# Two tiles of the first expert's early rows run beside the routing of the last batch, table look-ups moved ahead of a tile's waits, fewer zero rows stored late

## The reference, cut to what matters

```python
# attention: 4 batches x 8 heads = 32 heads, 576 rows, head size 64, with decay, causal
x = attention(q, k, v, f).transpose(...).reshape(2304, 512)
# mixture of 8 experts, each row goes to one expert
logits = normed(x) @ normed(expert_emb).T / tau
expert_idx, gate_w = argmax(logits), softmax(logits)[argmax]
for e in range(8):
    mask = expert_idx == e
    h = np.maximum(x[mask] @ w1[e], 0.0)             # 512 -> 1024
    out[mask] = gate_w[mask, None] * (h @ w2[e])     # 1024 -> 512
# dense part: w_in 512 -> 2048, softplus, w_out 2048 -> 512
out = softplus(out @ w_in) @ w_out
```

## Time and profile before

| | |
|---|---|
| median of 3 runs | 1006.88 us (1004.63 to 1007.55) |
| the profiled execution, its own time | 1005.88 us |
| its span, first to last instruction | 1004.0 us |
| mean granted TensorE clock | 0.976 of full |
| busy in the span | PE 950.3, DVE 564.8, ACT 399.2, POOL 321.3 us |

### The profile page before, as it was taken

One profiled execution on the slowest core, in us unless ns is written; L12 is line 12 of the kernel. 1 busy time (PEld: TensorE's weight loads), 2 busy tenths in 40 slices (PEclk: granted clock), 3 DMA queues, 4 the chain that ended last, 5 costly groups with the idle time before them and its releaser, 6 DMA issues.

```text
span 1004.0 us, 17301 instructions
## 1 busy us (share of the span) xinstructions
PE 950.3 (95%) x5536; PEld 827.0 (82%) x5537; DVE 564.8 (56%) x1153; ACT 399.2 (40%) x684; POOL 321.3 (32%) x169
## 2 busy tenths in 40 slices
PE   6999999999926999999999989999999999999997
PEld 4888888888815877887888778989989899899896
DVE  7566667787555556646666755344444434444433
ACT  6567667666431112302322133333333333333332
POOL 7355464353326334814777630010010100100101
PEclk9899999999968999999999999999999999999999
DMA  6664654484167153643666410010010000000000
GB/s 151 158 162 102 157 140 115 117 245 109 54 215 242 55 180 104 222 151 87 212 218 218 165 43 22 11 42 22 1 42 22 31 22 10 31 0 0 32 1 32
DMA packets 56011, 98.98 MB, mean 99 GB/s; under 512 B 23648, under 2 KB 23648, under 8 KB 55456
## 3 DMA queue, kind: packets, MB, share of 16 engines
q1 hardware_dynamic: 37440, 46.99, 17.9%
q10 hardware_dynamic: 15616, 41.96, 13.0%
q0 software_dynamic: 2912, 9.46, 2.5%
HBM read 81.14 MB, written 17.22 MB: 98 GB/s over the span
## 4 chain that ended last, share of the span: by engine, by line
PE 89%; DVE 5%; DMA 2%; issue 2%; POOL 1%; ACT 0%; POOLq 0%; DVEq 0%; SPq 0%; ACTq 0%
PE ps L1479 20%; PE ps L1492 19%; PE ps L1435 11%; PE ps L1414 11%; PE ps L1307 10%; PE ps L1268 7%; PE ps L1291 5%; PE ps L1324 2%; PE ps L1423 2%; DMA x_raw<-xs_dram 1%; DVE tile_meta L1131 1%; PE ps L1398 1%; PE ps L1269 1%; PE ps L1466 1%; DMA qk_raw<-qkT 0%
## 5 line engine op out<-in xcount | busy, mean ns | idle before, releaser
L1492 PE MATMUL ps<-W,ghl 128*128 128x512 f32 x864 | 215.4, 394 | 1.3 <-DVE ghl L1196 1.3
L522 POOL TENSOR_TENSOR W<-raw,W 128x2048 fp32r<-128x2048 f32 x36 | 165.2, 4615 | 141.7 <-ACT W L728 141.7
L1479 PE MATMUL ps<-yTh,W 128*128 128x384 f32 x768 | 198.7, 339 | 2.0 <-DVE yTl L1184 2.0
L1492 PEld LDWEIGHTS ps<-W,ghl 128*128 128x128 f32 x864 | 160.4, 188 | 32.1 <-DVE ghl L1196 1.6
L1190 DVE SCALAR_TENSOR_TENSOR sp_a<-ps,sp_a 128x384 f32<-128x384 f32 x96 | 53.5, 557 | 210.3 <-ACT sp_a L757 210.3
L728 ACT CAST W<-raw 128x2048 fp32r<-128x2048 f32 x36 | 67.1, 1909 | 222.5 <-PE ps L1414 88.9
L753 ACT ACTIVATE sp_a<-ps 128x384 f32<-128x384 f32 x96 | 47.3, 492 | 259.4 <-PE ps L1479 255.5
L1479 PEld LDWEIGHTS ps<-yTh,W 128*128 128x128 f32 x768 | 141.0, 189 | 9.2 <-issue 2.2
L557 POOL DMA_INDIRECT out<-out_sb,out_row x18 | 17.3, 960 | 380.9 <-DVE out_sb L1209 379.1
L1479 PE MATMUL ps<-yTl,W 128*128 128x384 f32 x384 | 130.1, 339 | 0.0
L1307 PE MATMUL ps<-v_ring,pT_sb 128*128 128x100 f32 (+1 forms) x960 | 119.5, 266 | 1.9 <-DVE lgh L867 1.9
(11 more groups left out here) (233 smaller groups left out, 1277.5 us busy)
## 6 DMA issues: line engine op xcount, KB each, us to landing
raw<-w ACTq DMA_DIRECT2D x28, 1024.0 KB, 6.5
qk_raw<-qkT SPq DMA_DIRECT2D x64, 288.0 KB, 4.5
x_raw<-xs_dram SPq DMA_DIRECT2D x22, 257.0 KB, 4.8
ys_dram<-y_sb SPq DMA_DIRECT2D x21, 256.5 KB, 5.9
y_raw<-ys_dram SPq DMA_DIRECT2D x18, 256.5 KB, 2.6
vT_ring<-vT SPq DMA_DIRECT2D x16, 288.0 KB, 4.4
v_ring<-v SPq DMA_DIRECT2D x32, 128.0 KB, 4.0
first_raw<-w ACTq DMA_DIRECT2D x4, 1024.0 KB, 5.6
```

The source lines that it names most:

```text
L522: pool.tensor_tensor(wcols(par, 1, c), RAW[c][:, :], wcols(par, 0, c).bitcast(F32), ALU.subtract).then_inc(wl_done, 1)
L1479: ins = pe.matmul(bank(f_ % 2, GN), W[:, a:a + P], y[par][:, c, :], start=(m == 0), stop=(m == 3 * DC - 1))
L1492: ins = pe.matmul(bank(2 + k), ghl[:, (f_ + 2) % 4, part, k * P:k * P + P], W[:, a:a + DM], start=(f_ == 0 and m == 0), stop=(f_ == FC2 - ...
```

## The change

1. **Early tiles.** Before the last batch is routed, SP loads the first 256 rows of expert 0's region into two buffers (`x_raws`). PE, DVE and ACT work them as tiles 0 and 1 with expert 0's weights. The rows' own tiles are taken out of the table: `early_rows` is the smaller of 256 and the rows that expert 0 has from the first three batches, and the remaining rows make tiles from 2 on. Tables and counts are longer by two. In these two tiles ACT, not DVE, takes the relu and the high part of the hidden values, and ACT scales the result of tile 0.
2. **Order on PE.** The two tiles' products are written in pieces among `ranks(LAST)` and the turns, in other PSUM banks. Half products of w1 have 12 matmuls, and w2 is cut into 12 + 12 for tile 0 and 12 + 6 + 6 for tile 1. The loop begins at tile 3.
3. **Look-ups.** All four look-ups of a pass of PE's loop stand at its head.
4. **Zeros.** Two zero stores for the first 256 rows are made near the start, ahead of the scatters. Late ones follow as before, but all seven others now stand ahead of `load_x(3)` in SP's queue.
5. 32 instead of 24 warm-up matmuls at the start. DVE's table code has a few more short operations.

The core of the diff (the rest is the same pieces written out for DVE and PE, the renamed buffers and the longer tables):

```diff
-TILES = NT // P + E - 1
+EARLY_TILES = 2
+TILES = NT // P + E - 1 + EARLY_TILES
...
+        EARLY_W1, EARLY_W2 = (0, 6), (5, 6)
+        WARM = 32
...
+            sp.wait_ge(zeros_set, 1)
+            for t in range(EARLY_TILES):
+                sp.dma_start(xs_dram[t * P:t * P + P, :], zeros[:, :]).then_inc(zeros_stored, 16)
...
+            sp.wait_ge(scattered, 16 * WHOLE)
+            sp.wait_ge(t_ready, 4 * (NH - 1))
+            for t in range(EARLY_TILES):
+                sp.dma_start(x_raws[t][:, :], xs_dram[t * P:t * P + P, :]).then_inc(early_loaded[t], 16)
...
+            early = sp.value_load(tab[0:1, TAB_EARLY:TAB_EARLY + 1], min_val=0, max_val=EARLY_TILES * P)
+            sp.wait_ge(xT_ready, EARLY_TILES)
+            sp.wait_ge(meta_read, EARLY_TILES)
             sp.wait_ge(scattered, 16 * NBLK)
-            sp.wait_ge(zeros_stored, 16)
-            sp.dma_start(x_raw[:, :], xs_dram[0:P, :]).then_inc(x_loaded, 16)
-            store_zeros([1, 2])
-            sp.wait_ge(tab_ready, 1)
-            sp.wait_ge(zeros_stored, 16 * 3)
-            load_x(1)
-            store_zeros(range(3, E))
-            load_x(2)
-            sp.wait_ge(zeros_stored, 16 * E)
+            sp.wait_ge(zeros_stored, 16 * (EARLY_TILES + 1))
+            sp.dma_start(x_raws[0][:, :], xs_dram[bass.ds(early, P), :]).then_inc(x_loaded, 16)
+            store_zeros(range(1, E))
...
+            sp.wait_ge(y_ready, 1)
+            sp.dma_start(ys_dram[0:P, :], y_sb[:, 0:DY]).then_inc(y_stored, 16)
+            sp.wait_ge(tab_ready, 1)
+            sp.wait_ge(zeros_stored, 16 * (EARLY_TILES + E))
+            load_x(3)
...
+            def early_relu(t):
+                act.wait_ge(mm1_done, t + 1)
+                if t > 0:
+                    act.wait_ge(hT_ready, t)
+                for half in range(2):
+                    ins = act.activation(h_sb[:, half * 512:half * 512 + 512], bank(EARLY_W1[t] + half), ACT.Relu)
+                ins.then_inc(relu_done, 1)
+
+            def early_hidden_high(t):
+                act.wait_ge(hT_ready, t + 1)
+                if t > 0:
+                    act.wait_ge(mm2_done, t)
+                for b in range(2):
+                    src = bank(2 + b).rearrange("p (c m) -> p c m", c=4)
+                    act.copy(hTh[:, 4 * b:4 * b + 4, :], src).then_inc(hh_done, 1)
+
+            early_relu(0)
             exps(LAST)
+            early_hidden_high(0)
+            early_relu(1)
+            act.wait_ge(meta_read, 1)
+            act.copy(y_sb[:, DM:DX], tile_meta[:, 0, :]).then_inc(meta_out, 1)
+            act.wait_ge(mm2_done, 1)
+            act.activation(y_sb[:, 0:DM], bank(EARLY_W2[0]), ACT.Copy, scale=tile_meta[:, 0, 1:2]).then_inc(y_ready, 1)
+            early_hidden_high(1)
...
+                if h == STEPS - 1:
+                    early_split(0)
+                    early_split(1)
                 dve_step(h, h)
...
+            early_meta(0)
+            early_meta(1)
...
+            then(nv.tensor_tensor(n_e[:, 0:1], n_e[:, 0:1], early_rows[:, 0:1], ALU.subtract))
...
+            def early_x_turn(t):
+
+                if t == 0:
+                    pe.wait_ge(ptD, 2 * NH)
+                pe.wait_ge(early_loaded[t], 16)
+                for c in range(DC):
+                    a = (4, 2)[t] * 512 + c * P
+                    ins = pe.transpose(ps[:, a:a + P], x_raws[t][:, c * P:c * P + P], ident[:, :])
+                ins.then_inc(xT_ready, 1)
+
+            def early_w1(t, half):
+
+                if half == 0:
+                    pe.wait_ge(wl_done, WL0)
+                    pe.wait_ge(xsplit, t + 1)
+                if t == 1 and half == 0:
+                    pe.wait_ge(x_ready, NH)
+                if t == 1 and half == 1:
+                    pe.wait_ge(rank_read, LAST + 1)
+                hi, lo = ((xTh, xTl), (xTh_early, xTl_early))[t]
+                n = 0
+                for c in range(DC):
+                    for x, low in ((hi, 0), (hi, 1), (lo, 0)):
+                        a = low * HALF + c * F1 + half * 512
+                        ins = pe.matmul(bank(EARLY_W1[t] + half), x[:, c, :], W[:, a:a + 512], start=(n == 0), stop=(n == 3 * DC - 1))
+                        n += 1
+                if half == 1:
+                    ins.then_inc(mm1_done, 1)
+
+            def early_w2(t, blocks):
+
+                if blocks[0] == 0:
+                    pe.wait_ge(hsplit, t + 1)
+                for c in blocks:
+                    for m, (x, low) in enumerate(((hTh, 0), (hTh, 1), (hTl, 0))):
+                        a = low * HALF + DC * F1 + c * DM
+                        ins = pe.matmul(bank(EARLY_W2[t]), x[:, c, :], W[:, a:a + DM], start=(c == 0 and m == 0), stop=(c == FC1 - 1 and m == 2))
+                if blocks[-1] == FC1 - 1:
+                    ins.then_inc(mm2_done, 1)
...
+                if h == STEPS - 1:
+                    early_x_turn(0)
+                    early_x_turn(1)
                 pe_step(h, h)
 
-            ranks(LAST)
...
+            early_w1(0, 0)
+            ranks(LAST)
+            early_w1(0, 1)
+            early_w1(1, 0)
+            h_turn(0)
+            early_w1(1, 1)
+            early_w2(0, range(0, 4))
+            h_turn(1)
+            early_w2(0, range(4, 8))
+            early_w2(1, range(0, 4))
+            x_turn(2)
+            early_w2(1, range(4, 6))
+            times_w1(2, 0, WL0)
             pe.wait_ge(tab_ready, 1)
             used = pe.value_load(tab[0:1, TAB_END + E - 1:TAB_END + E], min_val=OT, max_val=TILES)
-            x_turn(1)
-            h_turn(0)
-            times_w1(1, slot_of(1))
-            x_turn(2)
-            times_w2(0, slot_of(0))
-            with pe.Fori(2, used) as t:
+            x_turn(3)
+            early_w2(1, range(6, 8))
+            with pe.Fori(3, used) as t:
+                w, s, w_before, s_before = wait_of(t), slot_of(t), wait_of(t - 1), slot_of(t - 1)
                 h_turn(t - 1)
-                times_w1(t, slot_of(t))
+                times_w1(t, s, w)
                 x_turn(t + 1)
-                times_w2(t - 1, slot_of(t - 1))
+                times_w2(t - 1, s_before, w_before)
             last = pe.value_load(tab[0:1, TAB_LAST:TAB_LAST + 1], min_val=OT - 1, max_val=TILES - 1)
+            w_last, s_last = wait_of(last), slot_of(last)
```

More of the change, by code:

```diff
@@ L246, in build @@
         pos_ready, zrow_ready, tab_ready, shift_ready, scattered = sem("pos_ready"), sem("zrow_ready"), sem("tab_ready"), sem("shift_ready"), sem("scattered")
+        early_loaded = [sem(f"early_loaded{t}") for t in range(EARLY_TILES)]
         x_loaded, meta_read, meta_out = sem("x_loaded"), sem("meta_read"), sem("meta_out")
@@ L534, in _ @@
             pool.wait_ge(pos_ready, 1)
+            pool.wait_ge(zeros_stored, 16 * EARLY_TILES)
             scatter(range(0, 2 * NB))
@@ L542, in _ @@
             pool.wait_ge(pos_ready, 3)
+            for t in range(EARLY_TILES):
+                pool.wait_ge(early_loaded[t], 16)
             scatter(range(WHOLE, NBLK))
@@ L1121, in x_split @@
                 dve.wait_ge(xT_ready, t + 1)
-                if not (isinstance(t, int) and t < 1):
-                    dve.wait_ge(mm1_done, t)
+                dve.wait_ge(mm1_done, t)
                 nv.tensor_copy(xTh[:, :, :], src).then_inc(xh_done, 1)
@@ L1402, in entry, with wait_of, times_w1 @@
                 return pe.value_load(tab[0:1, bass.ds(t + at_, 1)], min_val=lo, max_val=hi)
-            def times_w1(t, slot):
-                pe.wait_ge(wl_done, WL0 if isinstance(t, int) and t < 1 else entry(TAB_WAIT, t, WL0 - 2, wl_count(E - 1, 1)))
+            def wait_of(t):
+                return entry(TAB_WAIT, t, WL0 - 2, wl_count(E - 1, 1))
+            def times_w1(t, slot, weights):
+                pe.wait_ge(wl_done, weights)
                 pe.wait_ge(xsplit, t + 1)
-                if not (isinstance(t, int) and t < 1):
-                    pe.wait_ge(relu_done, t)
+                pe.wait_ge(relu_done, t)
                 for half in range(2):
@@ L1424, in h_turn, with times_w2 @@
                 ins.then_inc(hT_ready, 1)
-            def times_w2(t, slot):
-                pe.wait_ge(wl_done, entry(TAB_WAIT, t, WL0 - 2, wl_count(E - 1, 1)) + 2)
+            def times_w2(t, slot, weights):
+                pe.wait_ge(wl_done, weights + 2)
                 pe.wait_ge(hsplit, t + 1)
-                if not (isinstance(t, int) and t < 1):
-                    pe.wait_ge(y_ready, t)
+                pe.wait_ge(y_ready, t)
                 n = 0
@@ L1518, in _ @@
             times_in(0, 0, 1)
-            times_w2(last, slot_of(last))
+            times_w2(last, s_last, w_last)
             group(0, 0, False)
```

89 lines of the change are left out of this document (53 added, 36 removed).

## The result

The changed kernel takes 978.66 us (median of four runs, 977.48 to 980.35), the kernel before 1006.5 us beside it. The ratio is 0.9725, 95% interval 0.9708 to 0.9742. 980.2 us was predicted, so the gain is 27.8 us where 26.7 were forecast (1006.88 to 980.2). The profiled execution took 978.26 us.

What follows compares the result with a forecast made beforehand. PE bounds the kernel, busy 950.3 of 1004.0 us, leaving idle time and half clock to win. Span 1004.0 - 24.7 (entry) - 2.0 (look-ups) = 977.3, plus 1.9 and 1.0 gives 980.2 us; range 971 to 989.

Steps and rivals of the forecast that it cites:

- the entry: Up to the loop's first w2 product: it begins at 329.8 instead of 354.46, gain 24.7 us, bounds 20 and 29.
- the loop: PE's loop behind its first w2 product: moved look-ups gain 2.0 us, bounds 0 and 2.6.
- The number of tiles: Tiles stored: 21 as before, no product added, the 96 matmuls of two tiles only moved.
- Into the attention's end: Early loads, PE's turns and DVE's splits fit into gaps at the attention's end, cost 0.
- Into the routing gap: Early products fill PE's 15.22 us idle; tile 0's w2 ends at 300.1, gate and scatters move 0.3 to 0.6.
- First new wait: Ahead of tile 1's w2, PE idles 2.5 us for hidden values that ACT writes behind tile 0's w2.
- Second new wait, the loop's start: Ahead of tile 3's turn, PE idles some 5 us for its load; turn at 317.5, bounds 313 and 322.
- both gates: Ahead of tile 3's load: zeros landed at 311.5, and DVE's copy for tile 2 ending at 308.5 or 313.
- Half clock behind the wait: Behind the wait for tile 3's load, half clock lengthens part of tile 3's w1 product by 1.2 us.
- Look-ups ahead of the first `h_turn`: At the loop's entry, four look-ups of about 3 us delay the first `h_turn`, costing 2.2 us.
- Look-ups in the loop: At the head of PE's loop passes, look-ups hide behind queued matmuls; gain 2.0 us, bounds 0 and 2.6.
- rival 1: At the loop's start, tile 3's load comes later still; 8 to 12 us less gain, 988 to 992, chance 0.12.

Runs made afterwards that it cites:

- e3: Changed kernel with tile 3's load ahead of the zero stores of experts 5 to 7 in SP's queue; 979.85 us, ratio 0.9734 to the kernel before.
- e2: Kernel before with only the look-ups moved as the change moves them; 1001.21 us, ratio 0.995 to the kernel before.
- e4: Changed kernel without the low parts of both early tiles' w2 products (32 of 48 matmuls); 982.5 us, ratio 0.9775 to the kernel before.
- e11: Changed kernel with one-column token and gate copies, x tiles at whole KB, tile 3's load ahead of experts 5 to 7's zeros; 985.87 us, ratio 0.9719.
- experiments 1 to 8: The runs e1 to e8, made on two chips with the kernel before beside them; ratios to it from 0.9722 to 0.995.
- e1: Changed kernel with the loop's look-ups back in their old places; 981.1 us, ratio 0.9763 to the kernel before.
- e7: Changed kernel with ACT's three DMA issues for expert 1's weights moved behind the last norms; 985.65 us, ratio 0.9804 to the kernel before.
- e5: Changed kernel with the split x tiles moved to whole KB addresses; 977.28 us, ratio 0.9722 to the kernel before.
- e6: Changed kernel with DVE's two-column token and gate copies made by a two-input instruction; 979.45 us, ratio 0.9743 to the kernel before.
- e8: Changed kernel with the edits of e3, e5 and e6 together; 978.3 us, ratio 0.9731 to the kernel before.
- e9: Changed kernel with each two-column token and gate copy made as two one-column copies; 981.65 us, ratio 0.9667 to the kernel before.
- e12: Changed kernel with the 24 warm-up products of the kernel before; 989.32 us, ratio 0.9747 to the kernel before.

## Why the prediction was right

The span was to shrink by 26.7 us and shrank by 27.5. At the first y turn the two kernels are 26.7 us apart (574.53 and 547.85), but by two misses that cancel: the entry gave 25.7 and not 24.7, the loop 1.0 and not 2.0. The last 0.8 us are luck. In the dense part the change moves two look-ups only, yet from its first product to the first of `w_out` it took 1.6 us less (11.83 against 13.40), because the kernel before had a stretch of half clock there. In the changed kernel such a stretch lay on the y turns and cost 0.8. The windows (length, busy, granted clock, DMA share, GB/s) of the kernel before, then two of the changed kernel:

```profile
579.00:584.00 5.00, 4.57 (x17) 0.66 0.00 0
```

```profile
547.00:553.00 6.00, 4.07 (x20) 0.72 0.13 47
553.00:558.00 5.00, 4.48 (x26) 1.00 0.00 2
```

That it is no work of the change is seen in e3, which has the changed kernel's code there and took 13.39 us. Of the other profiles e2, e4 and e11 took 11.8 and the rest 13.3 to 14.6. No run has the early tiles alone. Of the changed kernel's 27.8 us the look-ups alone made 4.4 in the kernel before (e2) and the warm-up at most 1.8. The rest, over 20 us, is left for the early tiles with their order of zeros, as the filled gap in the trace says.

- **The number of tiles** stayed at 21, and the matmuls of two tiles moved. Right.
- **Into the attention's end**: 0 predicted. The turns ran at 276.59 and 277.08, in the gap, and the value products behind them began at 277.86 instead of 277.35. The turns did not do that: the value products ahead of them already ran 0.5 us later (275.58 against 275.07). The attention's end varies by more than that among the versions of experiments 1 to 8 that have the change's attention (280.65 to 281.62).
- **Into the routing gap**: w2 of tile 0 was over at 301.3 where 300.1 was foretold. The order on PE was the one worked out. The table was ready at 299.2 against "about 298". Only the reason for the late exp was another. ACT's relu was over at 288.7, and the exp still waited 1.25 us for DVE, which had waited for the squares behind ACT's DMA issues, a term that the prediction had at nothing. In e1, e3 and e4, where those issues took 1.05 to 2.01 us, the exp came right behind the relu, at 288.33 to 288.54, near the 0.3 to 0.6 us of the prediction.
- **First new wait**: 2.65 us, 2.5 predicted. It is 2.64 or 2.65 in all ten other profiles with full products; e4's was 2.87.
- **Second new wait, the loop's start**: turn of tile 3 at 317.65, 317.5 predicted. The last zero was out at 307.93 and took 3.94 us (4 to 5 taken). The argument was right: it lay ahead of the weight loads, and e4 and e7 show what it costs when it does not. The 2.0 us that the prediction cites from the Trainium skill ("DMA: Bandwidth & Descriptors", Anatomy of one DMA — SWDGE (gpsimd) path) stand there for DMAs that GpSimd issues. SP's seven zeros took 2.79 to 3.94 us. PE waited 2.9 us there and not 5, since it had come later itself. In e1, e3, e5, e6 and e8 the held copy, not the zeros, set this turn, at 318.8 to 319.7 us. The prediction had both gates and reckoned from the zeros. It would have ended within 2 us either way, because they lie that close, but that it met 317.65 to 0.2 us is luck: the copy ended with a subtraction that was just over.
- **Half clock behind the wait**: 1.2 us were taken, none came in the profiled execution, whose clock was 1.00 from 32 us up to the y turns. In all eleven other profiles it came behind the first wait, for which the prediction took none, and in the eight with a wait of over 3 us ahead of tile 3's turn it came there too. As a price 1.2 us was right: from that turn to the loop's w2 e9, without half clock, took 10.2 us, e6 and e12, with the same addresses and with it, 11.2 and 11.3. The profile that the term was held against was the exception.
- **Look-ups ahead of the first `h_turn`**: 2.2 us, measured 1.29 of idle. The loop's w2 began at 328.74, 329.8 predicted: **gain 25.7 against 24.7**.
- **Look-ups in the loop**: 2.0, by e1 2.4 and by e2 3.5. But the stretch from there to the first y turn shrank by 1.0 us alone. **The term that was missing** is the address of the x tiles: 18 w1 products, each 0.1 us longer, took 1.3 to 1.8 us of it back (e5). From the kernel before to e1, which has the addresses and not the look-ups, the stretch grew by 1.4, and from e1 to the changed kernel it fell by 2.4. No view of the kernel before shows it. The diff does, in a line that looks like bookkeeping.
- **Rivals**: none came. e7 shows what rival 1 needs (the turn of tile 3 at 324.95, 7.3 us later, by one early burst of loads) and that its price of 8 us was sized right. e4 shows a rival that was not on the list: less work on PE, and a slower kernel.

## What to carry to other kernels

When tiles are run into a gap, read next what hands the following tile over. Here it was a queue of DMAs and a copy of two numbers, and making that copy one column at a time was worth 3.6 us (5.3 against e12). Work that hides in a wait is not free to remove: with 7 us less of it other transfers moved, the clock fell and the kernel lost 4 to 5 us. And a buffer that is moved is a change with a price of its own; after such a move, compare the spacing of one and the same instruction.

## What the runs showed of the hardware

- A matmul of a w1 product took 232 ns instead of 227 (median from start to start) when its x tiles (which it loads as weights) began 128 bytes behind a multiple of 2 KB. Whole KB were as fast as multiples of 2 KB.
- A VectorE copy of 128x2 between places of the local memory lasts up to 4.7 us beside a GpSimd subtraction (in the changed kernel and e3), one of 128x1 0.14 us (e9).
- A zero store of SP (257 KB) issued ahead of ACT's first 1 MB load for expert 2 landed in 2.8 to 3.9 us, one issued behind it in 6.2 to 10.5 us (ten profiles).
- A DMA issue of ACT took 0.4 us alone and up to 3.2 us for two in a row, with the DMA engines busy for 0.87 of the second one's 2.7 us (281.58 to 284.26 in the changed kernel). ACT's next square began only at its end.
- The clock stayed at full speed through waits of 2.65 and 2.91 us in one execution and fell to 1.2 GHz around the same 2.65 us in ten others (e1 has the same instructions ahead of it). Which of the two an execution gets was not in what this study could set. It may make a part of the 3 us and more that runs of one kernel differ by (e3 took 976.53 us at a mean granted clock of 0.993 and 981.25 at 0.988).
